# Expert and FFN up-projections as seven block products, one sequence after the other

## What is computed

```python
# attention, per head; block 32, window 16
k_sum = k.reshape(B, H, nb, block, D).max(axis=3)
v_sum = v.reshape(B, H, nb, block, D).mean(axis=3)
scores_l = scale * np.matmul(q, k.transpose(0, 1, 3, 2))   # kept where |i - j| < window
scores_s = scale * np.einsum('bhsd,bhnd->bhsn', q, k_sum) + np.log(block)
a = softmax(concatenate([scores_l, scores_s]))
attn_out = np.matmul(a, concatenate([v, v_sum]))
# experts, N = 1536 tokens; x is attn_out as [N, 512]
for e in range(E):
    h = np.maximum(x @ w1[e], 0.0)
    out += p[:, e:e + 1] * (h @ w2[e])
# feed-forward, on the experts' output
h = x @ w_in
g = h * (1.0 / (1.0 + np.exp(-1.702 * h)))
return g @ w_out
```

## Time and profile before

| | us |
|---|---|
| median of 3 runs | 878.36 |
| lowest, highest | 877.32, 1230.49 |
| the profiled execution, its span | 878.4 |
| TensorE busy in it | 855.3 |

### The profile page before, as it was taken

One profiled execution on the slowest core, in us unless ns is written; L12 is line 12 of the kernel. 1 busy time (PEld: TensorE's weight loads), 2 busy tenths in 40 slices (PEclk: granted clock), 3 DMA queues, 4 the chain that ended last, 5 costly groups with the idle time before them and its releaser, 6 DMA issues.

```text
span 878.4 us, 11397 instructions
## 1 busy us (share of the span) xinstructions
PE 855.3 (97%) x4224; PEld 709.1 (81%) x4224; DVE 248.8 (28%) x582; ACT 222.3 (25%) x494; POOL 226.6 (26%) x155
## 2 busy tenths in 40 slices
PE   5779999999999999999999999999999999999998
PEld 4668888888888888888888888888888888888886
DVE  4875412121212121212121211112333333333333
ACT  3665611112201012201022202032512133312121
POOL 2345712034502034502034502227510023300000
PEclk9999999999999999999999999999999999999999
DMA  9996350002200002200002200003200002010101
GB/s 213 234 227 150 110 213 0 1 5 97 90 1 0 0 24 96 72 0 0 0 24 96 72 0 0 0 0 119 73 0 0 0 24 72 1 48 0 48 0 48
DMA packets 41400, 47.34 MB, mean 54 GB/s; under 512 B 14944, under 2 KB 32416, under 8 KB 41248
## 3 DMA queue, kind: packets, MB, share of 16 engines
q1 hardware_dynamic: 39168, 45.94, 18.4%
q10 hardware_dynamic: 2208, 1.08, 0.6%
HBM read 42.76 MB, written 3.17 MB: 52 GB/s over the span
## 4 chain that ended last, share of the span: by engine, by line
PE 94%; DMA 4%; ACT 1%; DVE 0%; SPq 0%; issue 0%; ACTq 0%; POOL 0%; DVEq 0%; POOLq 0%
PE bank L761 30%; PE bank L762 30%; PE bank L763 30%; DMA v_win<-v_win 3%; PE bank L738 2%; PE bank L753 1%; PE bank L719 1%; DMA v_raw<-v_rows 1%; PE bank L729 1%; ACT prob L442 1%; SPq L269 0%; ACTq L456 0%; POOL q_bd L344 0%; ACT v_win L452 0%; DVE k_max L563 0%
## 5 line engine op out<-in xcount | busy, mean ns | idle before, releaser
L761 PE MATMUL bank<-x_hi,w_hi 128*128 (+1 forms) x576 | 225.7, 392 | 0.0
L762 PE MATMUL bank<-x_hi,w_lo 128*128 (+1 forms) x576 | 224.4, 390 | 0.0
L763 PE MATMUL bank<-x_lo,w_hi 128*128 (+1 forms) x576 | 224.2, 389 | 0.0
L626 DVE SCALAR_TENSOR_TENSOR h_lo<-bank,h_hi 128x512 fp32r<-128x512 f32 x96 | 66.4, 691 | 356.4 <-ACT h_hi L489 356.4
L761 PE MATMUL bank<-h_hi,w_hi 128*128 128x512 f32 x384 | 149.4, 389 | 0.0
L763 PE MATMUL bank<-h_lo,w_hi 128*128 128x512 f32 x384 | 149.4, 389 | 0.0
L762 PE MATMUL bank<-h_hi,w_lo 128*128 128x512 f32 x384 | 149.4, 389 | 0.0
L365 POOL TENSOR_TENSOR w_lo<-stage,w_hi 128x1024 fp32r<-128x1024 f32 x40 | 96.8, 2437 | 162.2 <-ACT w_hi L473 162.2
L489 ACT ACTIVATE h_hi<-bank 128x512 fp32r<-128x512 f32 x96 | 56.9, 592 | 313.9 <-PE bank L763 313.9
L391 POOL TENSOR_TENSOR x_acc<-x_acc,y_tmp 128x512 f32 (+1 forms) x48 | 60.5, 1297 | 262.1 <-DVE y_tmp L646 262.1
L761 PEld LDWEIGHTS bank<-x_hi,w_hi 128*128 128x128 f32 x576 | 108.1, 188 | 23.5 <-issue 0.8
(11 more groups left out here) (48 smaller groups left out, 601.7 us busy)
## 6 DMA issues: line engine op xcount, KB each, us to landing
stage<-weights SPq DMA_DIRECT2D x48, 512.0 KB, 3.3
v_win<-v_rows SPq DMA_DIRECT2D x8, 480.0 KB, 4.8
k_raw<-k_t SPq DMA_DIRECT2D x8, 384.0 KB, 6.4
q_bd<-q_t SPq DMA_DIRECT2D x16, 192.0 KB, 6.0
v_raw<-v_rows SPq DMA_DIRECT2D x8, 384.0 KB, 7.9
p_bc<-p_rows SPq DMA_DIRECT2D x1, 3072.0 KB, 9.9
out<-p_bc SPq DMA_DIRECT2D x12, 256.0 KB, 2.0
v_win<-v_win ACTq DMA_DIRECT2D x8, 132.0 KB
```

Source lines behind the costliest of these rows:

```text
L626: nc.vector.scalar_tensor_tensor(h_lo[:, f % NH, :], h_bank(cc, f)[:], 0.0, h_hi[:, f % NH, :].bitcast(F32), ALU.max, ALU.subtract).then_i ...
L761: nc.tensor.matmul(dst, w_h, a_h, start=first, stop=False)
L762: nc.tensor.matmul(dst, w_l, a_h, start=False, stop=False)
L763: return nc.tensor.matmul(dst, w_h, a_l, start=False, stop=last)
```

## The change

The token axis of each sequence is halved (384 columns, `HALF`), the 512 input features are halved into two blocks of 256, and hidden features are taken in pairs of 128. Such a step, four output blocks C11, C12, C21, C22 (hidden tile, token half) from 2 x 2 by 2 x 2 blocks, is done by seven products instead of eight. A product is 2 x 3 matmuls of 384 columns. Its weight side is one of four raw blocks or one of sums: GpSimd makes four sums of 256 columns per step (`sum_weights`), and seven blocks are split instead of four. Its activation side, the seven "moved" blocks `xb_hi`, `xb_lo`, is made once per phase. There are four phases: experts on sequence 0 (16 steps), experts on sequence 1 (16), FFN on sequence 0 (8), FFN on sequence 1 (8), 48 steps in all. `refill` marks the last step of a phase, in which the next phase's seven blocks are split (`high_part` on ScalarE, `low_moved` on VectorE and GpSimd) while the step runs.

Products accumulate in three PSUM banks: P1, then P6, P7 and P4 on top of it, in `ps_x`; P2 in `ps_y`; P5, then P3, in `ps_z`. ScalarE's `keep` copies `ps_x` after P1, P6 and P7 into `snap`, and VectorE's `add_c11`, `add_c22`, `add_c12` add a snapshot to get a C block. A hidden tile is then gated (for experts the ReLU and the probability in one operation, written to PSUM), and split. The 8 output tiles of the step before stand between the products (`down`), and VectorE's `take_y` adds each to `xa` in SBUF. Weights are loaded and split in every step, for each sequence anew.

Attention's groups 0 to 11 (sequence 0) run ahead of the steps; groups 12 to 23 run one in a step, in steps 0 to 11 (their values one step later). Keys and values now come from HBM as windows, values also as columns (summed by VectorE, turned by one matmul, spread by a ScalarE copy). The output is written features first and transposed on the host.

```diff
+MOE_STEPS = EXPERTS * PAIRS_E
+STEPS = BATCH * (MOE_STEPS + PAIRS_2)
+FFN0 = BATCH * MOE_STEPS
+FIRST = (0, MOE_STEPS, FFN0, FFN0 + PAIRS_2)
+LAST = (MOE_STEPS - 1, FFN0 - 1, FFN0 + PAIRS_2 - 1, STEPS - 1)
...
+ORDER = ("P1", "P2", "P5", "P6", "P7", "P4", "P3")
+MOVED = {"P1": 0, "P2": 1, "P5": 2, "P6": 3, "P7": 4, "P4": 5, "P3": 6}
+HELD = {"P1": 0, "P2": 1, "P4": 2, "P5": 3, "P6": 4, "P7": 5, "P3": 6}
+NP = len(ORDER)
...
+            def sum_weights(g):
+                a11, a12, a22, a21 = (stage[:, g % 2, BW * i:BW * (i + 1)] for i in range(4))
+                pool.wait_ge(stage_in[g % 2], 16 * (g // 2 + 1))
+                wait_count(pool, sumlo_done, g)
+                nc.gpsimd.tensor_tensor(w_sum[:, 0, :], a21, a22, ALU.add).then_inc(wsum_step, 1)
+                nc.gpsimd.tensor_tensor(w_sum[:, 2, :], a11, a21, ALU.subtract).then_inc(wsum_step, 1)
+                pool.wait_ge(wsum_step, 4 * g + 1)
+                nc.gpsimd.tensor_tensor(w_sum[:, 1, :], w_sum[:, 0, :], a11, ALU.subtract).then_inc(wsum_step, 1)
+                pool.wait_ge(wsum_step, 4 * g + 3)
+                nc.gpsimd.tensor_tensor(w_sum[:, 3, :], a12, w_sum[:, 1, :], ALU.subtract).then_inc(wsum_step, 1)
...
+            def keep(g, n):
+                act.wait_ge(up_done, made(g, ("P1", "P6", "P7")[n]))
+                if g:
+                    act.wait_ge(c_done, 3 * (g - 1) + (1, 3, 2)[n])
+                nc.scalar.activation(snap[:, n, :], ps_x, ACT.Copy).then_inc(snap_done, 1)
...
+            def sigmoid(g, c):
+                at = {"C11": ps_y, "C22": snap[:, 2, :], "C21": ps_x, "C12": ps_z}[c]
+                n = READY[c]
+                if c == "C21":
+                    act.wait_ge(up_done, made(g, "P4"))
+                else:
+                    act.wait_ge(c_done, 3 * g + {"C11": 1, "C22": 2, "C12": 3}[c])
+                wait_count(act, gated_done, 4 * g + n - 2)
+                nc.scalar.activation(sig[:, n % 2, :], at, ACT.Sigmoid, scale=1.702).then_inc(sig_done, 1)
+            def high_hidden(g, c):
+                at = {"C11": ps_y, "C22": ps_y, "C21": ps_x, "C12": ps_z}[c]
+                act.wait_ge(gated_done, 4 * g + READY[c])
+                wait_count(act, y_done, 8 * (g - 1))
+                nc.scalar.activation(h_hi[:, g % 2, TILE[c], :], at, ACT.Copy).then_inc(hhi_done, 1)
...
+            for g in range(STEPS):
+                ph, ffn, more = phase_of(g), g >= FFN0, g + 1 < STEPS
+                refill = g in LAST[:3]
+                keep(g, 0)
+                if more:
+                    high_raw(g + 1)
+                if refill:
+                    high_part(act, ph + 1, 0)
+                if ffn:
+                    sigmoid(g, "C11")
+                high_hidden(g, "C11")
+                for k in step_group(g):
+                    exponent(k)
+                for k in step_group(g - 1):
+                    take_x(k)
+                if more:
+                    high_sums(g + 1, 0)
+                if refill:
+                    high_part(act, ph + 1, 1)
+                keep(g, 1)
+                if more:
+                    high_sums(g + 1, 1)
+                if refill:
+                    high_part(act, ph + 1, 2)
+                keep(g, 2)
+                if g % GROUPS == 0 and KT + g // GROUPS < UNITS:
+                    value_means(KT + g // GROUPS)
+                if refill:
+                    high_part(act, ph + 1, 3)
+                if ffn:
+                    sigmoid(g, "C22")
+                high_hidden(g, "C22")
+                if ffn:
+                    sigmoid(g, "C21")
+                high_hidden(g, "C21")
+                for k in step_group(g):
+                    copy_prob_t(k)
+                if more:
+                    high_down(g + 1, 0)
+                    high_down(g + 1, 1)
+                if refill:
+                    high_part(act, ph + 1, 4)
+                    high_part(act, ph + 1, 5)
+                if ffn:
+                    sigmoid(g, "C12")
+                high_hidden(g, "C12")
+                if refill:
...
+            def low_moved(ph, i):
+                dve.wait_ge(xhi_done, high_parts(ph, i))
+                nc.vector.tensor_tensor(xb_lo[:, i, :, :], moved_source(ph, i), xb_hi[:, i, :, :].bitcast(F32),
+                                        ALU.subtract).then_inc(xlo_dve, 1)
...
+            def add_c11(g):
+                dve.wait_ge(up_done, made(g, "P2"))
+                dve.wait_ge(snap_done, 3 * g + 1)
+                nc.vector.tensor_tensor(ps_y, ps_y, snap[:, 0, :], ALU.add).then_inc(c_done, 1)
+            def add_c22(g):
+                dve.wait_ge(up_done, made(g, "P5"))
+                dve.wait_ge(snap_done, 3 * g + 3)
+                dve.wait_ge(hlo_done, 4 * g + 1)
+                nc.vector.tensor_tensor(snap[:, 2, :], ps_z, snap[:, 2, :], ALU.add).then_inc(c_done, 1)
+            def add_c12(g):
+                dve.wait_ge(up_done, made(g, "P3"))
+                nc.vector.tensor_tensor(ps_z, ps_z, snap[:, 1, :], ALU.add).then_inc(c_done, 1)
...
+            def gate(g, c):
+                n = READY[c]
+                at = {"C11": ps_y, "C22": ps_y, "C21": ps_x, "C12": ps_z}[c]
+                of = {"C22": snap[:, 2, :]}.get(c, at)
+                if c == "C21":
+                    dve.wait_ge(up_done, made(g, "P4"))
+                else:
+                    dve.wait_ge(c_done, 3 * g + {"C11": 1, "C22": 2, "C12": 3}[c])
+                if g < FFN0:
+                    q = g // PAIRS_E
+                    dve.wait_ge(p_in[q % 2], 16 * (q // 2 + 1))
+                    half = int(c[2]) - 1
+                    nc.vector.scalar_tensor_tensor(at, of, 0.0, p_bc[:, q % 2, HALF * half:HALF * (half + 1)],
+                                                   ALU.max, ALU.mult).then_inc(gated_done, 1)
+                else:
+                    dve.wait_ge(sig_done, 4 * (g - FFN0) + n)
+                    nc.vector.tensor_tensor(at, of, sig[:, n % 2, :], ALU.mult).then_inc(gated_done, 1)
+            def low_hidden(g, c):
+                at = {"C11": ps_y, "C22": ps_y, "C21": ps_x, "C12": ps_z}[c]
+                dve.wait_ge(hhi_done, 4 * g + READY[c])
+                nc.vector.tensor_tensor(h_lo[:, g % 2, TILE[c], :], at, h_hi[:, g % 2, TILE[c], :].bitcast(F32),
...
+            for g in range(STEPS):
+                ph, refill = phase_of(g), g in LAST[:3]
+                if g:
+                    take_y(g - 1, 0)
+                    low_hidden(g - 1, "C12")
+                for k in step_group(g):
+                    mask_scores(k)
+                add_c11(g)
+                if g:
+                    take_y(g - 1, 1)
+                gate(g, "C11")
+                if g:
+                    take_y(g - 1, 2)
+                low_hidden(g, "C11")
+                if refill:
+                    low_moved(ph + 1, 1)
+                if g:
+                    take_y(g - 1, 3)
+                for k in step_group(g):
+                    invert_sums(k)
+                if g:
+                    take_y(g - 1, 4)
+                add_c22(g)
+                if g:
+                    take_y(g - 1, 5)
+                gate(g, "C22")
+                gate(g, "C21")
+                if refill:
+                    low_moved(ph + 1, 3)
+                if g:
+                    take_y(g - 1, 6)
+                low_hidden(g, "C22")
+                low_hidden(g, "C21")
+                if refill:
+                    low_moved(ph + 1, 5)
+                add_c12(g)
+                if g:
+                    take_y(g - 1, 7)
+                gate(g, "C12")
+                if refill:
+                    low_moved(ph + 1, 6)
...
+            def product(g, name):
+                ph, i = phase_of(g), MOVED[name]
+                if g in FIRST:
+                    if i in POOL_LOW:
+                        pe.wait_ge(xlo_pool, len(POOL_LOW) * ph + POOL_LOW.index(i) + 1)
                     else:
...
+                        pe.wait_ge(xlo_dve, len(DVE_LOW) * ph + DVE_LOW.index(i) + 1)
+                if name == "P1":
+                    pe.wait_ge(rawlo_done, g + 1)
+                    wait_count(pe, hlo_done, 4 * (g - 1) + READY["C21"])
+                    if g == 0:
+                        pe.wait_ge(masked_done, B_GROUPS)
+                elif name == "P2":
+                    wait_count(pe, hlo_done, 4 * (g - 1) + READY["C22"])
+                    if g == 0:
+                        pe.wait_ge(x_done, B_GROUPS)
+                elif name == "P5":
+                    pe.wait_ge(sumlo_done, g + 1)
+                    wait_count(pe, hlo_done, 4 * g)
+                    if g == 0:
+                        pe.wait_ge(vmean_done, KT)
+                elif name == "P6":
+                    pe.wait_ge(snap_done, 3 * g + 1)
+                elif name == "P7":
+                    pe.wait_ge(snap_done, 3 * g + 2)
+                elif name == "P4":
```

(61 more changed lines are left out.)

841 lines of the change are left out of this document (418 added, 423 removed).

## The result

The changed kernel takes 899.47 us (median; 897.99 to 901.10), the kernel before 877.86: the ratio is 1.0242, with a 95% interval of 1.0217 to 1.0267. The forecast was 854.1 and faster; it is slower. The profiled execution has a span of 897.6 us; a run's time is 1.8 us above its span. The forecast started from the span before (878.4), so I compare it with the span. (One of the four times of the kernel before, 1230.49, lies far off the other three, 877.3 to 878.4.)

A forecast was written before the change was run, and what follows sets the result against it. TensorE bounds the kernel. Start 51, step 0's 7 + 1, products 746.9, attention 23.9 + 4, FFN 5, refills 12 and end 3.3 sum to 854.1 us; forecast's own range 846 to 864, whole range 836 to 884.

The forecast's parts named there:

- The price of a matmul: Products on TensorE: 172.9 ns per matmul of 384 columns, 4320 matmuls, 746.9 us, 34.9 us less than before.
- a plain step: Loop step without attention: 15.56 us, all engines fit, no stall, with 0.2 us to spare at the next P1.
- Rival 3: Weight load as floor: no matmul starts before its load's 188 ns are over; +65 us, about 919; chance 0.07.
- rival 4: The 12.9 ns belong to the old loop; unrolled matmuls take nearly column time, 798 to 820 us; chance 0.05.
- rival 1: Fewer costs: 169.7 ns a matmul gives 840 us, 836 with the start at 47 as well; chance 0.20.
- The attention in the steps: Second sequence's 12 groups inside steps 0 to 12: 23.9 us of TensorE plus 4 us of waits; steps of 17.8.
- the start: Before step 0: last unit's queries after 39 to 42 us of loads, P1 at about 51 us, range 45 to 57.
- step 0: First step: 7 us lost to x's splits and group 12's chain, 1 more for a stretch at half clock.
- the phase changes: Refill steps 15, 31, 39: splitting the next phase's blocks delays P1 by 0.7 us and P5 by 3; 12 us in all.
- the contention: VectorE and GpSimd excluding each other in SBUF during refills: 4 x 3 x 0.8 = 10 us, only in the range.
- FFN steps: 16 FFN steps: ScalarE's sigmoid and high-part order makes low C21 late, 0.3 us each, 5 us, to 9.
- Rival 2: More waits: collisions in refills and attention steps (+10), FFN steps (+5), PSUM writes (5); 865 to 885 us; chance 0.22.

## Why the prediction was wrong

**Right.** The price of a matmul (172.9 ns against 173.3), hence 746.9 us of products (748.7); a plain step (15.56 against 15.60) without a stall; a step with attention (17.8 against 17.78). Rival 3 (the weight load as the floor, 188 ns) and rival 4 (the 13 ns as the loop's, 160) both fell by the 173.3, and rival 1's 169.7 with them. The attention in the steps was 4 us dearer than the forecast's, nearly all of it in the three steps with key maxima and value sums (19.25 instead of 17.78).

**The step that failed first: the start, 51 us.** It was made of bytes over a rate, "39 to 42 us" for the last unit's queries, as if the queue issued all loads at once. The rows of before allowed that: there the DMA engines were full for 72 us. After the change they were not; the loads stood behind a wait for a buffer. I had asked how many bytes, not what each issue waits for, and which issues stand behind it. Another order of the queue with a free place for unit 2's keys is shown to be worth 11.6 of the 17.3 us; 5.7 stay open. The range of the term, 45 to 57, didn't hold it. (The 27480 packets that the forecast gives as all are those under 8 KB; in all there are 27488, which changes nothing.)

**The second: step 0, 7 us lost.** The walk followed x's blocks through VectorE and ScalarE and the group through its chain, but not the snapshots, which stand behind high C11 and the exponents on ScalarE. It was 8.1 us more. Moving the snapshots gives 2.8 of them back. Taking the attention out shortens the step by 5.4, some 1.3 of it being matmuls that the forecast had. The walk also had the low parts at 0.97, and two took 1.98 and 1.49. How much of the rest is the half clock (0.71 and 0.70 in the windows from 60 to 100 us) isn't separated.

**The third: the phase changes, 12 us.** The mechanism was right in the main: low C21 and low C12 behind the low parts of the next phase, P1 and P5 waiting. The size was 23.1. The walk had P1 0.7 us late, and it was 2.55 to 2.59; it had no wait of P7 in the last step (0.95 to 1.68), and nothing in the step before (0.5, 0.5 and 1.2). It had VectorE's low parts at 0.97, and at the first two changes three of the four took 1.7 to 2.1. I had worked the contention out at 10 us, put it in the range and left it out of the sum without a reason. With it the term would have been 22, but that would have been luck: without the low parts' contention only some 3 us came back, while another order of the same work gave 8.6.

**FFN steps**, 0.3 each, were 0.47: 2.5 us over all of them (one of them, step 32, is in the 23.1 as well).

Together: 17.3 + 8.1 + 4.0 + 14.3 = 43.7 us, of the 43.5. So the products take 33 us less than before (781.8 less 4320 x 0.1733), and the change lost that again, and some 20 us more, mostly in waits ahead of step 1 and at the phase changes. Rival 2 named more waits and stopped at 885, because it held no term for the start; its dearer writes to PSUM fell, since the gates that write there take 559 ns against 556 for `take_y`, which writes to SBUF. That the time came out slower bears out no rival: rival 3, the only slower one, had another mechanism. No rival held a longer start, though the queue's waits for buffers could be listed from the code.

## What to carry to other kernels

For a prologue, don't divide bytes by a rate: write down for each DMA issue which buffer it waits for, and what stands behind it in the same queue. When work becomes shorter than the time that it used to hide, every short chain (snapshots, low parts, gates) has to be put in the order of its deadline; here such orders, with one more place for keys, turned 2.4% slower into 0.7% under the kernel before, which is no clear difference. And a contention that the trace shows belongs in the sum wherever the new code has the same pair of operands, but as a longer operation in the walk, not as a count times its price: whether it costs anything depends on what stands behind it.

## What was not expected of the hardware

**A stretch of half clock costs nothing in front of a wait, and 1.6 us behind it.** Step 40 took 19.24 us in the changed kernel and 20.81 in the run with the snapshots moved. P1 starts there after the same idle time (2.58 and 2.55 us). In the changed kernel the clock falls at once, while P5 is going to wait anyway; in the other run it stays whole, P5 waits 2.96 instead of 1.46 us, and the clock falls behind that. The windows of the changed kernel, then of the other run, P1 starting at 754.50 and at 751.52:

```profile
754.00:757.00 3.00, 2.50 (x8) 2.53 (x9) 2.27 (x3) 1.06 (x2) 3.00 (x2) 0.55 0.00 0
...
761.00:764.00 3.00, 2.14 (x12) 2.17 (x13) 2.21 (x5) 1.08 (x3) 2.89 (x3) 1.00 0.00 0
```

```profile
751.00:754.00 3.00, 2.48 (x14) 2.51 (x15) 2.27 (x3) 1.08 (x2) 3.00 (x2) 1.00 0.00 0
...
761.00:764.00 3.00, 3.00 (x13) 3.00 (x13) 1.02 (x2) 0.60 (x2) 0.00 (x0) 0.62 0.00 0
```

The run with `take_y` 6 moved has the second pattern too (P5 waits 3.40 us, then the clock falls), with 21.04 us, and so has step 32 of the run with the 16 extra matmuls, with 19.93 instead of 18.37. An edit far away can so cost or give 1.6 us.

**VectorE's held-up low parts end 0.8 us behind GpSimd's operation.** In step 15 GpSimd's ends at 352.03 and VectorE's low part at 352.85; at 359.04 and 359.85; at 362.07 and 362.89 (from the rows above): 0.81 to 0.82 us each time, for an operation of 0.96 by itself. So they ran, nearly whole, one after the other and not side by side. The Trainium skill ("SBUF — State Buffer", "Who interferes with whom") says so of a VectorE instruction with two SBUF inputs, and these rows agree. GpSimd's own operations are longer there as well: its low part takes 2.16 us and 1.85 in step 0, and L452 takes 2.63 and 2.41 on average.
